# An FFT filter and two three-pass MLPs on one core: weight sums moved into the transform and through device memory

## The reference

```python
X = np.fft.rfft(x, axis=1)
Y = X * (filt_r + 1j * filt_i)[None]
x = np.fft.irfft(Y, n=3008, axis=1).reshape(6016, 256)
h = x @ moe_w_in;  g = np.maximum(0.01 * h, h);  x = g @ moe_w_out
h = x @ moe2_w_in; g = np.maximum(h, 0.0) ** 2;  y = g @ moe2_w_out
```

## Time and profile before

| | |
|---|---|
| median of 3 executions | 1152.91 us (1152.83 to 1155.33) |
| profiled execution, its own time | 1154.74 us |
| its span in the trace | 1153.0 us |
| mean granted clock of TensorE | 0.989 of full |
| busy: PE, DVE, ACT, POOL | 1110.2, 898.8, 556.5, 317.2 us |

### The profile page before, as it was taken

One profiled execution on the slowest core, in us unless ns is written; L12 is line 12 of the kernel. 1 busy time (PEld: TensorE's weight loads), 2 busy tenths in 40 slices (PEclk: granted clock), 3 DMA queues, 4 the chain that ended last, 5 costly groups with the idle time before them and its releaser, 6 DMA issues.

```text
span 1153.0 us, 14228 instructions
## 1 busy us (share of the span) xinstructions
PE 1110.2 (96%) x5312; PEld 935.5 (81%) x5312; DVE 898.8 (78%) x1191; ACT 556.5 (48%) x973; POOL 317.2 (28%) x228
## 2 busy tenths in 40 slices
PE   6999969999999999999999998999999999999997
PEld 6998947788888888888888877788888888888886
DVE  1787668888788788788788888787887887887774
ACT  2354535455445455454455655354454454554443
POOL 0356457622022122201213587211211220210000
PEclk9899989999999999999999999899999999999999
DMA  9655020000000000000011100000000000000000
GB/s 226 178 164 168 24 73 0 1 1 1 1 1 1 1 1 1 0 1 1 0 47 56 46 0 1 1 37 1 21 17 1 35 1 1 37 0 1 37 1 34
DMA packets 16852, 35.12 MB, mean 30 GB/s; under 512 B 2064, under 2 KB 6288, under 8 KB 16784
## 3 DMA queue, kind: packets, MB, share of 16 engines
q1 hardware_dynamic: 16640, 34.02, 9.7%
q10 hardware_dynamic: 144, 0.20, 0.1%
HBM read 28.05 MB, written 6.16 MB: 30 GB/s over the span
## 4 chain that ended last, share of the span: by engine, by line
PE 78%; DVE 9%; ACT 4%; POOL 3%; issue 3%; DMA 1%; SPq 1%; DVEq 0%
PE PS L745 13%; PE PS L746 12%; PE PS L747 12%; PE PS L753 11%; PE PS L755 11%; PE PS L754 11%; DVE GL L598 2%; PE PS L676 2%; PE PS L664 2%; DVE GF L590 2%; DVE GF L592 2%; ACT GH L442 2%; DMA X<-in_x 1%; PE PS L697 1%; PE PS L653 1%
## 5 line engine op out<-in xcount | busy, mean ns | idle before, releaser
L598 DVE TENSOR_TENSOR GL<-GF,GH 128x512 fp32r<-128x512 f32 (+1 forms) x384 | 287.9, 752 | 165.2 <-ACT GH L442 152.2
L442 ACT ACTIVATE GH<-GF 128x512 fp32r<-128x512 f32 (+1 forms) x384 | 238.5, 621 | 297.6 <-DVE GF L592 149.4
L745 PE MATMUL PS<-GH,WOH 128*128 128x512 f32 (+1 forms) x768 | 298.7, 389 | 8.8 <-DVE GL L598 8.8
L746 PE MATMUL PS<-GL,WOH 128*128 128x512 f32 (+1 forms) x768 | 297.6, 387 | 0.0
L747 PE MATMUL PS<-GH,WOL 128*128 128x512 f32 (+1 forms) x768 | 297.2, 387 | 0.0
L753 PE MATMUL PS<-XH,WIH 128*128 128x512 f32 (+1 forms) x672 | 262.3, 390 | 17.6 <-DVE GF L583 9.9
L755 PE MATMUL PS<-XH,WIL 128*128 128x512 f32 (+1 forms) x672 | 260.3, 387 | 0.0
L590 DVE SCALAR_TENSOR_TENSOR GF<-GF 128x512 f32<-128x512 f32 (+1 forms) x192 | 179.5, 955 | 3.3
L745 PEld LDWEIGHTS PS<-GH,WOH 128*128 128x128 f32 x768 | 144.8, 189 | 41.4 <-DVE GL L598 13.8
L592 DVE SCALAR_TENSOR_TENSOR GF<-GF 128x512 f32<-128x512 f32 (+1 forms) x192 | 171.4, 913 | 4.7 <-ACT GF L436 1.3
L747 PEld LDWEIGHTS PS<-GH,WOL 128*128 128x128 f32 x768 | 144.7, 188 | 28.0
(11 more groups left out here) (55 smaller groups left out, 1043.7 us busy)
## 6 DMA issues: line engine op xcount, KB each, us to landing
FL<-in_filt SPq DMA_DIRECT2D x32, 224.0 KB, 3.5
TB<-in_tab SPq DMA_DIRECT2D x32, 182.0 KB, 2.8
X<-in_x SPq DMA_DIRECT2D x22, 256.0 KB, 8.7
out_y<-YT SPq DMA_DIRECT2D x4, 1024.0 KB, 4.3
WIF<-in_w1i SPq DMA_DIRECT2D x8, 256.0 KB, 4.0
WOF<-in_w1o SPq DMA_DIRECT2D x8, 256.0 KB, 4.9
WIF<-in_w2i SPq DMA_DIRECT2D x8, 256.0 KB, 2.6
WOF<-in_w2o SPq DMA_DIRECT2D x8, 256.0 KB, 2.9
```

Of the source, the lines that this page charges most:

```text
L442: nc.scalar.activation(GH[:, g, 0:width(s)], GF[:, g, 0:width(s)], ACT.Copy).then_inc(g_hi[kind], 1)
L598: nc.vector.tensor_tensor(GL[:, g, 0:w], GF[:, g, 0:w], GH[:, g, 0:w].bitcast(f32), ALU.subtract).then_inc(g_lo[kind], 1)
L745: nc.tensor.matmul(acc, wh, xh, start=first, stop=False)
L746: nc.tensor.matmul(acc, wh, xl, start=False, stop=False)
```

## The change

1. All sums of the first MLP's weights are made in the transform: blocks 0, 1, 4 and 5 in pieces between POOL's unit additions (tables `WI_SUM`, `WI_HI`, `WI_LO`), 2 and 3 at unit 16, 6 and 7 after unit 31, before the sums of the first pair. The raw loads are issued earlier (`WI_LOAD`).
2. The first pair's rounding and rests are made in pieces of one column block, spread over chunks 15 to 20 (`x_round0`, whose third piece waits on ACT for the third operation of `x_forms(0)`). The third and second operation of `x_forms` change places.
3. The last three chunks (21 to 23, `FILL` = 21) move to slots 0 and 1, between the products, with their sums in PS banks 4 and 5.
4. The second MLP's weight sums and splits are made in slots 8 to 39, in 32 pieces (`CHUNKS`), one for each slot. A piece is loaded to a small buffer, summed on POOL, rounded on ACT, split on POOL and stored high and low in device memory (`wi2`, `wo2`). From slot 41 finished blocks are loaded into WIH, WIL, WOH and WOL.
5. Snapshots 1 and 7 go to their block's place in GF (which needs the `down` of the block six earlier), the order of ACT and DVE in a slot changes, and the last slot has the order of the others.

```diff
+        WI_LOAD = {0: 0, 2: 1, 6: 2, 9: 3, 12: 4, 14: 5, 20: 6, 23: 7}
+        WI_SUM = {3: (0, 0), 4: (0, 1), 5: (1, 0), 6: (1, 1), 18: (4, 0), 19: (4, 1), 20: (5, 0), 21: (5, 1)}
+        WI_HI = {5: 0, 7: 1, 20: 4, 22: 5}
+        WI_LO = {7: (0, 0), 8: (0, 1), 9: (0, 2), 10: (1, 0), 11: (1, 1), 12: (1, 2),
+                 22: (4, 0), 23: (4, 1), 24: (4, 2), 25: (5, 0), 26: (5, 1), 27: (5, 2)}
+        FILL = 2 * CH - 3
+        CHUNKS = 4 * KU
...
+            for j in range(CHUNKS):
+                i, h = j // 2, j % 2
+                if j == 0:
+                    sp.wait_ge(p1_ps, 1)
+                else:
+                    sp.wait_ge(pw_out, 32 * j)
+                if j < 2 * KU:
+                    sp.dma_start(PWF[:, 0:4, :], w2i[:, i, :, 64 * h:64 * h + 64]).then_inc(pw_raw, 16)
+                    sp.wait_ge(pw_lo, j + 1)
+                    sp.dma_start(wi2[:, i, 0, :, 64 * h:64 * h + 64], PWH[:, :, :].bitcast(f32)).then_inc(pw_out, 16)
+                    sp.dma_start(wi2[:, i, 1, :, 64 * h:64 * h + 64], PWL[:, :, :].bitcast(f32)).then_inc(pw_out, 16)
+                else:
+                    i -= KU
+                    sp.dma_start(PVF[:, :], w2o[:, i, D * h:D * h + D]).then_inc(pw_raw, 16)
+                    sp.wait_ge(pw_lo, j + 1)
...
             for k in range(KU + 1):
                 if k < KU:
                     sp.wait_ge(p3_ps, last1 + k + 1)
-                    sp.dma_start(WIF[:, k, 0:4, :], w2i[:, k, :, :]).then_inc(wi_raw[k], 16)
+                    sp.dma_start(WIH[:, k, :, :].bitcast(f32), wi2[:, k, 0, :, :]).then_inc(wi_raw[k], 16)
+                    sp.dma_start(WIL[:, k, :, :].bitcast(f32), wi2[:, k, 1, :, :]).then_inc(wi_raw[k], 16)
...
+            def w2_sums(j):
+
+                f = [PWF[:, i, :] for i in range(7)]
+                pool.wait_ge(pw_raw, 16 * (j + 1))
+                nc.gpsimd.tensor_tensor(f[4], f[3], f[2], ALU.add).then_inc(pw_s, 1)
...
+            for k in (6, 7):
+                for part in range(2):
+                    wi_sums(k, part)
+            for k in (6, 7):
+                for part in range(3):
+                    wi_split(k, part)
             x_forms(0)
-            x_split(0)
+            x_split(0, 2)
+            x_split(0, 3)
...
+            for p in range(1, NP - 1):
+                for k in range(KU):
+                    j = KU * (p - 1) + k
+                    if j < 2 * KU:
+                        w2_sums(j)
+                    if 2 <= k < 6:
+                        x_split(p + 1, k - 2)
+                    w2_split(j)
+                    if k == 1:
+                        x_forms(p + 1)
...
+            def w2_round(j):
+                if j < 2 * KU:
+                    act.wait_ge(pw_s, 4 * j + 4)
+                    nc.scalar.activation(PWH[:, :, :], PWF[:, :, :], ACT.Copy).then_inc(pw_hi, 1)
+                else:
+                    act.wait_ge(pw_raw, 16 * (j + 1))
+                    nc.scalar.activation(PVH[:, :], PVF[:, :], ACT.Copy).then_inc(pw_hi, 1)
...
+            for c in range(CH, FILL + 1):
                 turned_back(c)
-                if c >= 2 * CH - 4:
-                    x_round(0, c - (2 * CH - 4))
+                if c in (CH + 1, CH + 2):
+                    wi_round(c - CH + 5)
+                if CH + 3 <= c < CH + 7:
+                    x_round0(c - CH - 3)
+                if c == CH + 7:
+                    x_round(0, 2)
+                if c == CH + 8:
+                    x_round(0, 3)
+                if c == FILL:
+                    wo_round(0)
+                    wo_round(1)
...
             for s in range(SLOTS + 1):
+                if s >= 1:
+                    g_round(s - 1, UB)
                 if s < SLOTS:
                     snap1(s)
-                if s >= 1:
-                    g_round(s - 1, UB)
...
-                if p == 0 and k + 3 < KU:
-                    wi_round(0, k + 3)
-                late = 1 if p == 0 else 0
+                late = 2 if p == 0 else 0
                 if 0 <= k - 2 - late <= 3 and p < 2 * NP - 1:
                     x_round(p + 1, k - 2 - late)
-                if KU * (NP - 1) + 6 <= s < KU * (NP - 1) + 6 + KU:
-                    wi_round(1, s - KU * (NP - 1) - 6)
-                if KU * (NP - 1) + 7 <= s < KU * (NP - 1) + 7 + KU:
-                    wo_round(1, s - KU * (NP - 1) - 7)
+                if KU <= s < KU + CHUNKS:
+                    w2_round(s - KU)
...
+                elif first:
+                    pe.wait_ge(y_sb, 2 * CH)
+                    pe.wait_ge(v_sb, 2 * CH)
...
+            for s in range(SLOTS):
                 group_a(s)
+                if s == 0:
+                    fill(FILL)
                 down(4 * s - LAG)
                 if s >= 1:
                     group_d(s - 1)
+                if s == 1:
+                    fill(FILL + 2)
                 down(4 * s - LAG + 1)
                 group_b(s)
+                if s == 0:
+                    fill(FILL + 1)
```

More of the change, by code:

```diff
@@ L103, in fft_mlp_kernel @@
         wi_s = sem("wi_s")
+        pw_raw = sem("pw_raw")
+        pw_s = sem("pw_s")
+        pw_hi = sem("pw_hi")
+        pw_lo = sem("pw_lo")
+        pw_out = sem("pw_out")
         wi_hi = sem("wi_hi")
@@ L227, in _, with wi_sums @@
             nc.gpsimd.memset(XF[32:IM, :, :, :], 0.0).then_inc(xf_pad, 1)
-            def wi_forms(mlp, k):
-                n = 4 * (mlp * KU + k)
+            WI_STEPS = {k: 4 * n for n, k in enumerate((0, 1, 2, 3, 4, 5, 6, 7))}
+            def wi_sums(k, part):
+                n = WI_STEPS[k]
                 f = [WIF[:, k, i, :] for i in range(7)]
[L233 to L239, removed]
@@ L299, in _ @@
+            for k in (6, 7):
+                for part in range(2):
+                    wi_sums(k, part)
+            for k in (6, 7):
+                for part in range(3):
+                    wi_split(k, part)
             x_forms(0)
-            x_split(0)
+            x_split(0, 2)
+            x_split(0, 3)
             for k in range(KU):
-                wo_split(0, k)
-                if k + 3 < KU:
-                    wi_forms(0, k + 3)
-                    wi_split(0, k + 3)
-                if k == 1:
-                    x_forms(1)
-                if k == 5:
-                    x_split(1)
@@ L310, in _ @@
[L310 to L325 removed]
+                wo_split(k)
@@ L327, in n1_out @@
+            for p in range(NP, 2 * NP):
+                x_forms(p)
+                for i in range(4):
+                    x_split(p, i)
         def n1_out(c, half):
@@ L609, in _ @@
                 if s < SLOTS:
-                    g_split(s, UA)
+                    g_act(s, UA)
+                if s == 0:
+                    sequence(FILL)
                 if s >= 1:
@@ L737, in _ @@
             pe.wait_ge(u_sb, UNITS)
-            for c in range(CH - 1, 2 * CH):
-                if c + 1 < 2 * CH:
-                    turn_back(c + 1)
+            for c in range(CH - 1, FILL):
+                turn_back(c + 1)
                 sequence(c)
@@ L818, in down, with fill @@
                 mm.then_inc(down_ps, 1)
-            for s in range(SLOTS - 1):
+            def fill(c):
+                if c + 1 < 2 * CH:
+                    turn_back(c + 1)
+                sequence(c)
+            for s in range(SLOTS):
                 group_a(s)
+                if s == 0:
+                    fill(FILL)
                 down(4 * s - LAG)
@@ L829, in _ @@
                 down(4 * s - LAG + 3)
-            s = SLOTS - 1
-            group_a(s)
-            group_d(s - 1)
-            down(4 * s - LAG)
-            group_b(s)
-            down(4 * s - LAG + 1)
-            group_c(s)
-            down(4 * s - LAG + 2)
-            group_d(s)
-            for n in range(4 * s - LAG + 3, 4 * SLOTS):
+            group_d(SLOTS - 1)
+            for n in range(4 * SLOTS - LAG, 4 * SLOTS):
                 down(n)
```

232 lines of the change are left out of this document (143 added, 89 removed).

## The result

The changed kernel takes 1138.1 us (median, 1135.3 to 1139.1); the kernel before took 1152.9 beside it. The ratio is 0.986, with an interval of 0.984 to 0.989: 14.8 us faster, where 7.2 were forecast. Run again beside other kernels it took 1136.3 us (0.984 to 0.988). The sign was right and the time lies in the range; the amount was off by a factor of two.

A forecast was written before the change was run, and what follows sets the result against it. PE, busy 1110 of 1153 us, was taken as the bound, with some 32 us to win. Gains of 24.6 less losses of 16.3 (ring) and 1.1 (DVE) gave -7.2 us: 1146 against the median 1152.9, range 1128 to 1186.

The forecast's parts named there:

- Unit 16 and the pieces between units: Transform: PE's 1.8 us wait after unit 16 goes; pieces fit POOL's idle time at no cost; three loads cost 0.3 us.
- rival 4: Transform: loads before unit 16 stall the units by 0.5 us each, +1.5 us; no chance of its own given.
- Slots 0 and 1: Start of the products: first product at 141.2 us, first down at 157.2, not 165.0; gain 7.8 us, unit 16's included.
- Rival 3: Slots 0 and 1: new waits take back the 7.8 us, 1154, no change; near-even chance 0.11, shared with a 10.9 us turn.
- Rest of the first pair: Slots after 0 and 1: no ACT wait for weight sums, POOL's long operations spread; gain 4.0 of 4.3 us.
- Change of MLPs: Between the MLPs: finished weights are loaded six slots ahead of use; gain 11.2 of 11.4 us.
- Last slot: End of the kernel: gain 1.6 us.
- The ring: Slots 8 to 23: turns of 10.4 us, 180 us against 161, less 4.3 ACT can be late, plus 1.6: loss 16.3 us.
- my likeliest case: Whole kernel: a ring turn of 9.7 to 10.7 us puts the time between 1133 and 1150; chance 0.38.
- My sign of being wrong: Ring stores: issue to landing takes 4 us; the forecast is wrong if that differs by 1 us either way.
- Rival 1: Ring stores: 32 ns a piece, not 16; turn 2.3 us longer, 1183; slower 0.36, of which 0.24 up to 1186.
- Rival 2: Slots 8 to 23: turn of 8.9 us, only x_split slots stick out, loss about 1 us, time 1130; chance 0.15.

The follow-up runs named there:

- e9: Changed kernel with w2_split ahead of x_split, x_forms(0) ahead of the splits of blocks 6 and 7, last chunk's copy early, snap1 in its own buffer; 1122.6 us.
- e3: Changed kernel with the stores of the first 16 pieces in runs of 128 bytes, not 256 (output not the reference's); 1142.8 us, ratio 0.991.
- e8: Changed kernel with snap1 in a buffer of its own (SA) instead of its place in GF; 1133.4 us, ratio 0.984.
- e10: Changed kernel with DVE's old order in the second MLP: activation A ahead of whole_c, split A ahead of activations D and C; 1138.1 us, ratio 0.987.
- e5: Changed kernel with x_forms(0) put ahead of POOL's six splits of weight blocks 6 and 7; 1132.2 us, ratio 0.981.
- e6: Changed kernel with DVE's copy of the last chunk moved ahead of slot 1's activations and splits; 1135.0 us, ratio 0.984.
- e2: Changed kernel with the first 16 pieces stored in runs of 1792 bytes, not 256, and four late loads a block, not two; 1131.9 us, ratio 0.982.

## Why the prediction was right in sign and wrong in amount

- *Unit 16 and the pieces between units.* Right: 2.0 us for 1.8. Between the starts of inverse 16 and 17 the lead grows from 0.05 to 2.01 us, and by the same 2.0 in every run, so this isn't chance. With 0.05 us before it, the pieces and the three loads cost nothing (rival 4 fell).
- *Slots 0 and 1.* 5.0 us at slot 2 for 7.8; 7.5 in the second run, of which 1.2 had come before inverse 16. Rival 3 (no earlier first product) fell. The chain was right at each step, and the times came 0.9 us (first product) and 1.4 us (first `down`) late. "I give both the same loss by the clock" was the weak sentence. PE ran at half clock (0.50) for 6.8 us, from inside the stall in front of the first `down` on, in the kernel before (first line) and in the changed one (second); in its second run (third line) it was 3.4 us, from the end of the stall on:

```profile
161.00:167.80 6.80, 4.22 (x10) 3.35 (x11) 6.21 (x9) 4.18 (x8) 4.34 (x5) 0.50 0.00 0
...
157.40:164.20 6.80, 5.56 (x13) 4.43 (x14) 2.45 (x4) 0.40 (x1) 5.50 (x5) 0.50 0.17 50
...
157.20:160.60 3.40, 3.40 (x8) 2.71 (x9) 0.00 (x0) 0.00 (x0) 3.32 (x3) 0.52 0.00 0
```

  Before, 2.8 us of it lay behind the start of the first `down` (165.0); in the change 5.6 (from 158.6), and half of the difference is the 1.4 us by which the lead falls from the first `down` to slot 2. In the second run it is 3.4 us and the lead falls by 0.3. An idle stretch that is shortened doesn't give back all of itself while the slow clock behind it stays, and how long it stays differed between two executions of one kernel. In e9 no window between 130 and 1117 us is below full clock.
- *Rest of the first pair.* 5.1 us for 4.0: right. *Change of MLPs.* 10.7 for 11.2: right; the late loads were in time. *Last slot.* 2.1 for 1.6: right.
- *The ring: this step failed.* The term was 16.3 us, with 1.1 for DVE beside it; measured were 5.7 and 5.1, and nothing for DVE. The mechanism, its place and its waits were as written, and the turn was mis-sized: 9.5 us in plain slots for 10.4, because of the four additions (1.4 to 1.7 us for 2.0 in most plain turns), the stores with their handover (3.5 for 3.9) and the split (1.15 for 1.3). At 10.4 us every slot loses; at 9.5 those with an `x_split` do, and the plain ones repay. The six turns with 1024 columns of `x_split` take 11.1 to 12.8 us, where I had 12.4. The two that meet `x_forms`, which I had not priced, take 11.4 and 10.0.

  The 14 turns that begin in slots 9 to 22 take 150.9 us in all, and my terms give 159.2. The seven turns in slots 9 to 15 take 75.1 us (first additions at 242.4 and 317.5) against slots of 10.2 us, 3.7 us too long, which the 4.3 us of tolerance absorb but for 0.9 of them. The six that follow take 66.7 us (to 384.2), and there slots are only 9.8 us long, since that pair is 480 columns wide (10.1 and 9.9 in its first two): some 7.6 us too long, and by slot 24 PE has lost 4.8. I had worked out both pairs with 161 us for 16 slots and one tolerance; the second pair is where the loss is. With a turn of 9.5 us my own sum gives 165.6 - 161 - 4.3 + 1.6 = 1.9 us, not 5.7: the mis-sized turn made it too large and the single tolerance too small, and part of the two errors cancelled. So it is luck that 1138 lies in the 1133 to 1150 of my likeliest case, whose turn was 9.7 to 10.7 us. My sign of being wrong, the time of the stores, could not catch it either: from the first issue to both landed and the load issued it was 3.5 us for 3.9, well within the 1 us that I allowed.
- *Rival 1 (small runs cost double)* fell: 17.8 ns for 251 bytes, against the 32 it needs. In e3, with 128 bytes, packets are cheaper still, at 13.9 ns, and only their number makes the store longer. The Trainium skill ("DMA: Bandwidth & Descriptors", Specifications) asks for 512 bytes at least for full rate and names no factor for less; the double was my reading of it. The rule holds here in that the bytes of a small run are dear (0.071 ns a byte at 251 bytes, from 17.8 / 251; 0.042 at 1920 bytes, from the earlier trace rows), but no doubling of a packet below 512 bytes shows in any run.
- *Rival 2 (hidden ring)* was nearer than I gave it credit for: its turn of 8.9 us is 0.6 below what was measured, the forecast's 10.4 is 0.9 above, and its time of 1130 is as far from 1138 as the forecast's 1146.
- *Not foreseen:* 2.0 us in slots 56 to 94. Shown: it sits in four stalls at changes of pairs, DVE's activations beside `x_forms` take 4.7 us there for three, and the wait of the first snapshot is worth 0.5 to 0.6 of it (e8, and e9 the same with 1.5 left). DVE's old order doesn't take it away (e10). What the rest comes from is open: ACT's new order is only argued, and neither that nor a later start of `x_forms` was tried.

The sum: gains 24.6 forecast, 22.9 measured and 25.5 in the second run (5.0 or 7.5, 5.1 or 5.2, 10.7 or 10.8, 2.1, without rounding); losses 17.4 forecast, 7.7 and 7.2 measured. Slots 24 to 48 give another 0.4. The error is in the losses; the gains were 1.7 us short or 0.9 over. Two slips in the working are small: the places where PE loses time add up to 30.1 us by their own numbers, not 32, and by the earlier trace rows the fixed part of the load is 2.6 - 4 x 0.165 = 1.94 us, not 1.85.

## What to carry to other kernels

A buffer that goes round once per slot costs nothing as long as a turn fits in the slot, and beyond that its excess, less what the engines can be late; so work that isn't part of the turn (here one `x_split` of 2.4 us on POOL) belongs behind the step that releases the DMA, never ahead of it: changing its place gave back 5.6 us of 5.7. When a forecast hangs on a threshold, work out each turn against the length of its own slot, the narrow ones apart, and let the chances follow how near the threshold is; here 0.9 us in a turn of 9.5 was the step from 1.9 to 16.3 us in the sum. Where PE waits on a list that runs in order, ask of each item ahead who needs it first (e5); moving one item past work that PE needs just behind it (e6) only moves the stall.

## What the runs showed of the hardware

- A DMA packet took 13.9 ns at 142 bytes and 17.8 at 251; the 1920 and 4096 bytes of the earlier trace rows lie on nearly the same line, with no step between. In e2, where runs of 256 and 1792 bytes are mixed, the mean packet of 723 bytes took 35.8 ns (16.8% of 16 engines in 163 us, 12240 packets); the line through the first two gives 34.7.
- Two stores of 224 KB issued one after the other and the load behind them took 5.0, 5.9 and 6.5 us together with runs of 1792, 256 and 128 bytes: seven times as many packets cost 0.9 us, fourteen times as many 1.5.
- POOL's addition of 128 x 64 took 0.32 us in some turns and 0.6 to 0.8 in others, its split of 448 columns 1.15 or 1.6; that it is DVE's work beside it that makes the difference was not tried. An activation on DVE of 0.66 us (480 columns) or 0.69 (512) took 1.31 or 1.77 to 1.79 while POOL made its sums of 512 columns.
- Executions that are alike differ by up to 4 us at unit 17, before any of the edits acts, and the granted clock differs there: 0.50 from 27.7 to 34.5 us in the change, with PE busy 5.9 of 6.8 us; in e9 the mean over the first 130 us is 1.00. Such differences stay in the total. The two windows, of the changed kernel and of e9:

```profile
27.70:34.50 6.80, 5.94 (x28) 5.90 (x29) 0.41 (x1) 1.69 (x3) 0.00 (x0) 0.50 1.06 299
```

```profile
0.00:130.00 130.00, 120.52 (x930) 113.30 (x931) 87.37 (x126) 60.76 (x108) 75.10 (x93) 1.00 0.64 177
```
